# Two-token score levels, weight halves and output banks in the opening of a linear-attention and MLP kernel

## The reference

```python
f = 1.0 / (1.0 + np.exp(-f_logit))
for t in range(S):
    state = f[:, :, t, :, None] * state + np.einsum('bhd,bhe->bhde', k[:, :, t], v[:, :, t])
    y[:, :, t] = np.einsum('bhd,bhde->bhe', q[:, :, t], state)
# x = y as tokens x 384, then
xn = (x - mu) / np.sqrt(var + 1e-06) * g_ln
x = x + np.maximum(xn @ w_ch1, 0.0) @ w_ch2
# then relu(x @ w_in), a convolution over three tokens, h * sigmoid(conv), @ w_out
```

## Time and profile before

| | |
|---|---|
| median of 3 runs | 773.96 us (771.0 to 778.25) |
| the profiled execution, device time | 777.86 us |
| its span, first to last instruction | 776.1 us |
| TensorE matmul busy | 700.0 us (90%) |
| VectorE busy | 558.6 us (72%) |
| ScalarE busy | 309.0 us (40%) |
| GpSimd busy | 222.9 us (29%) |
| mean granted clock of TensorE | 0.979 |

### The profile page before, as it was taken

How to read it: one execution, slowest core, us unless ns; L and a number is a source line. 1 busy time by engine, 2 the same in 40 slices (tenths; PEclk the granted TensorE clock), 3 DMA queues, 4 the chain that set the end, 5 groups by cost and what they waited for, 6 DMA issues and landing times.

```text
span 776.1 us, 19962 instructions
## 1 busy us (share of the span) xinstructions
PE 700.0 (90%) x8672; PEld 653.0 (84%) x8672; DVE 558.6 (72%) x998; ACT 309.0 (40%) x590; POOL 222.9 (29%) x204
## 2 busy tenths in 40 slices
PE   1345689879999999999999899999989999999998
PEld 1245688779899999899899899999989999999997
DVE  6978888757776976876885886452458767767765
ACT  2353132033034134125125114212367766776764
POOL 7667632205324524434432631430000000000000
PEclk9999999789899999999999999999999999999999
DMA  8652511174134324414406220204220201201000
GB/s 249 199 164 63 113 57 49 53 154 114 52 74 150 87 55 128 129 37 140 134 3 174 59 98 32 87 17 156 89 87 1 70 20 52 71 29 42 36 36 35
DMA packets 23223, 65.82 MB, mean 85 GB/s; under 512 B 4288, under 2 KB 15296, under 8 KB 23136
## 3 DMA queue, kind: packets, MB, share of 16 engines
q1 hardware_dynamic: 23136, 64.55, 28.7%
HBM read 55.09 MB, written 9.45 MB: 83 GB/s over the span
## 4 chain that ended last, share of the span: by engine, by line
PE 59%; DVE 15%; DMA 10%; POOL 8%; issue 4%; SPq 2%; ACT 1%; DVEq 0%; POOLq 0%; ACTq 0%
DMA NEAR<-near 9%; PE bank L1145 9%; PE bank L1147 8%; PE bank L1146 8%; PE bank L952 8%; PE bank L954 7%; PE bank L953 7%; PE bank L884 6%; DVE AT L761 3%; DVE Q L738 3%; DVE TOT L732 2%; POOL NEAR L566 2%; DVE A L773 2%; POOL NEAR L581 2%; POOL NEAR L568 2%
## 5 line engine op out<-in xcount | busy, mean ns | idle before, releaser
L884 PEld LDWEIGHTS bank<-Q,K 48*64 48x64 f32 x3840 | 70.4, 151 | 52.5 <-issue 52.4
L657 ACT ACTIVATE HHI<-bank 128x384 fp32r<-128x384 f32 x96 | 47.0, 491 | 168.8 <-PE bank L954 168.6
L884 PE MATMUL bank<-Q,K 48*64 48x32 f32 x3840 | 75.3, 234 | 42.0 <-DVE Q L738 30.8
L1122 DVE SCALAR_TENSOR_TENSOR TB<-HB,CW,TB 128x440 f32<-128x440 f32 x112 | 75.8, 677 | 47.0 <-ACT TB L1085 45.0
L952 PE MATMUL bank<-HHI,W2H 128*128 128x384 f32 x288 | 105.6, 367 | 0.0
L952 PE MATMUL bank<-XH,W1H 128*128 128x384 f32 x288 | 103.3, 359 | 0.6 <-DVE XL L831 0.6
L954 PE MATMUL bank<-HHI,W2L 128*128 128x384 f32 x288 | 99.0, 344 | 0.0
L953 PE MATMUL bank<-HLO,W2H 128*128 128x384 f32 x288 | 98.7, 343 | 0.0
L953 PE MATMUL bank<-XL,W1H 128*128 128x384 f32 x288 | 97.3, 338 | 0.2 <-issue 0.2
L954 PE MATMUL bank<-XH,W1L 128*128 128x384 f32 x288 | 97.3, 338 | 0.0
L836 DVE SCALAR_TENSOR_TENSOR HLO<-bank,HHI 128x384 fp32r<-128x384 f32 x96 | 53.1, 554 | 47.1 <-ACT HHI L657 46.1
(11 more groups left out here) (116 smaller groups left out, 1443.0 us busy)
## 6 DMA issues: line engine op xcount, KB each, us to landing
NEAR<-near SPq DMA_DIRECT2D x23, 960.0 KB, 4.9
V<-v SPq DMA_DIRECT2D x8, 576.0 KB, 9.0
x2d<-X SPq DMA_DIRECT2D x8, 576.0 KB, 4.3
F<-f SPq DMA_DIRECT2D x14, 288.0 KB, 5.3
K<-k SPq DMA_DIRECT2D x14, 288.0 KB, 5.1
Q<-q SPq DMA_DIRECT2D x14, 288.0 KB, 6.6
XB<-x2d SPq DMA_DIRECT2D x6, 663.0 KB, 5.5
out<-OB SPq DMA_DIRECT2D x6, 660.0 KB, 4.4
```

Source lines behind the costliest of these rows:

```text
L657: nc.scalar.activation(HHI[:, g % RA], ub[g % 2][:, 0:T], ACT.Relu).then_inc(hh_ready, 1)
L884: ins = mm(scores[half, par, at:at + QUARTER], K[u.par][rows, c, j, half], right[:, :, 1, :], start=True, stop=True)
L1122: nc.vector.scalar_tensor_tensor(out=TB[:, g % RB], in0=HB[:, g % RB, tap:tap + TB_], scalar=CW[:, g, tap:tap + 1], in1=TB[:, g % RB], op0 ...
```

## The change

The first unit no longer uses NEAR, and the low halves of the weights no longer come from GpSimd.

- **Two-token blocks of unit 0.** `even` and `odd` are two more score levels: K with the even tokens of Q before the gates are applied, and, after K's even tokens are scaled (`baseK`), with the odd ones. `self` puts them into AT with a predicated copy. `baseK` and `baseQ` of unit 0 now wait for them. `near`, `nsum` and `neary` of unit 0 are gone, and so are three loads of 960 KB.
- **Weights.** ScalarE scales and rounds in one pass (`whi`). For the pieces 0 to 7 TensorE forms in each half of a piece (128x384) diag(g_ln) times the staged half (an fp32 product) minus the high half (an fp32r product) in one of the two banks of `up` (`wsub`), and ScalarE copies it out (`wlo`). The pieces 8 to 11 are done by VectorE in one pass (`wlv`).
- **Banks.** For unit 0 `y`, `kv` and `xnt` write the banks 0, 1 and 2, and `xadd` of unit 0 is a copy on ScalarE without an addition.
- **State.** ST has two buffers; `sscale` reads one and writes the other, and so waits for the `y` of the chunk before instead of its own.
- **Setup.** GpSimd makes one more mask (SELF) and clears AT[0] earlier and AT[1] too.
- **Order.** START and LOADS are new lists.

```diff
-        ST = attn("ST", [P, NP, 2 * D])
+        ST = [attn(f"ST{i}", [P, NP, 2 * D]) for i in range(2)]
+        NPE = 8
...
             def load_w(_, j):
                 if j >= NS:
-                    sp.wait_ge(wl_ready, j - NS + 1)
+                    if j - NS < NPE:
+                        sp.wait_ge(wp_done, 2 * (j - NS + 1))
+                    else:
+                        sp.wait_ge(wd_ready, j - NS - NPE + 1)
...
-            def weights(_, j):
-                _, hi, lo = WJ[j]
-                pool.wait_ge(wh_ready, j + 1)
-                nc.gpsimd.tensor_tensor(lo, stage(j), hi.bitcast(F32), ALU.subtract).then_inc(wl_ready, 1)
...
-                    nc.scalar.activation(stage(j), stage(j), ACT.Copy, scale=GLN[:, kt:kt + 1]).then_inc(wg_ready, 1)
-                    act.wait_ge(wg_ready, j + 1)
-                nc.scalar.copy(WJ[j][1], stage(j)).then_inc(wh_ready, 1)
+                    nc.scalar.activation(WJ[j][1], stage(j), ACT.Copy, scale=GLN[:, kt:kt + 1]).then_inc(wh_ready, 1)
+                else:
+                    nc.scalar.copy(WJ[j][1], stage(j)).then_inc(wh_ready, 1)
+
+            def wlo(_, h):
+                act.wait_ge(wp_done, h + 1)
+                nc.scalar.copy(half_of(WJ[h // 2][2], h), ub[h % 2][:, 0:DM]).then_inc(wl_ready, 1)
...
+            def wsub(_, h):
+                j = h // 2
+                if h == 0:
+                    pe.wait_ge(gd_ready, 1)
+                pe.wait_ge(wh_ready, j + 1)
+                if h > 1:
+                    pe.wait_ge(wl_ready, h - 1)
+                by = GD[:, j // (F1 // WCH)] if j < NW1 else ID[:]
+                to = ub[h % 2][:, 0:DM]
+                mm(to, by, half_of(stage(j), h), start=True, stop=False)
+                mm(to, MINUS, half_of(WJ[j][1], h), start=False, stop=True).then_inc(wp_done, 1)
...
             def baseK(p, _):
+                if u.first:
+                    dve.wait_ge(even_done[p.ahead], 1)
...
             def sscale(u, c):
-                dve.wait_ge(y_done, u.count(NC, c + 1))
-                if c or not u.first:
+                if c == (1 if u.first else 0):
+                    dve.wait_ge(prep_ready[0], u.count(PREPS, PREPS))
+                if u.index or c:
+                    dve.wait_ge(y_done, u.count(NC, c))
                     dve.wait_ge(st_ready, u.count(NC, c))
...
                     if c == 0 and u.half == 0:
-                        ins = nc.vector.memset(st, 0.0)
+                        if u.first:
+                            dve.wait_ge(const_ready, 2)
+                        ins = nc.vector.memset(to, 0.0)
...
             def up(u, g):
                 if u.first:
-                    pe.wait_ge(wl_ready, NW1)
+                    pe.wait_ge(wl_ready, 2 * NPE)
```

More of the change, by code:

```diff
@@ L309, in phase_a @@
                 "xh", "xl")
-        TREE = ("gates", "baseK", "baseQ", "pT", "pK", "pQ", "score", "mask", "copy")
+        TREE = ("gates", "even", "odd", "self", "baseK", "baseQ", "pT", "pK", "pQ", "score", "mask", "copy")
         PERIOD = steps("""
@@ L353, in phase_a @@
[L353 to L357, removed]
@@ L408, in wstage, with nears, bank_of, state @@
             return WST[j % 2][:, 0:flat].rearrange("p (a b) -> p a b", a=n)
-        def near_of(u, c):
-            return NEARS[1] if u.first and c == 1 else NEARS[0]
+        def nears(u, more):
+            return u.count(NC, more - NC)
+        def bank_of(kind, u):
+            return {"y": bank[0], "kv": bank[1], "xnt": bank[2]}[kind] if u.first else yb
+        def state(u, c):
+            return ST[(u.index * NC + c) % 2]
         def stage(j):
@@ L682, in xb @@
                     nc.scalar.copy(nxt.XBH[0][:, d], nxt.XB[0][:, d]).then_inc(nxt.xbh_ready, 1)
[L684 to L685 removed]
+            walk(act, dict(wb=wb, xb=xb, gates=gates, near=near_, copy=copy, xadd=xadd, ktok=ktok, xh=xh, hhi=hhi,
+                           xout=xout, diag=diag, whi=whi, wlo=wlo))
         def vector(dve):
@@ L849, in xb @@
                                             ALU.subtract).then_inc(nxt.xbl_ready, 1)
-            walk(dve, dict(wb=wb, xb=xb, baseK=baseK, baseQ=baseQ, pK=pK, pT=pT, pQ=pQ, mask=mask, nsum=nsum, xadd=xadd,
-                           sscale=sscale, st=st_, norm=norm, xn=xn, xl=xl, hlo=hlo))
+            walk(dve, dict(wb=wb, xb=xb, baseK=baseK, baseQ=baseQ, self=self_, wlv=wlv, pK=pK, pT=pT, pQ=pQ,
+                           mask=mask, nsum=nsum, xadd=xadd, sscale=sscale, st=st_, norm=norm, xn=xn, xl=xl, hlo=hlo))
         def tensor(pe):
@@ L862, in score @@
                 pe.wait_ge(prep_ready[p.ahead], u.count(PREPS, st + 1))
+                if st == 0 and u.first:
+                    pe.wait_ge(self_done[p.ahead], 1)
                 if st > MASKED:
@@ L888, in ktr @@
             def ktr(u, c):
-                if c:
+                if u.first and c or u.index == 1 and c == 0:
+                    pe.wait_ge(ktok_ready, u.count(NC, c))
+                elif c:
                     pe.wait_ge(st_ready if c == 1 else xl_ready, u.count(NC, 1))
@@ L901, in y @@
             def y(u, c):
-                first = c == 0 and u.half == 0
-                pe.wait_ge(ktok_ready, u.count(NC, c + 1))
+                first, to, before = c == 0 and u.half == 0, bank_of("y", u), state(u, c - 1)
+                if not u.first:
+                    pe.wait_ge(ktok_ready, u.count(NC, c + 1))
+                elif c:
+                    pe.wait_ge(x_ready, c)
                 if u.first and c == 0:
@@ L977, in down @@
                 ins.then_inc(down_done, 1)
-            walk(pe, dict(score=score, ktr=ktr, y=y, kv=kv, xnt=xnt, xacc=xacc, up=up, down=down))
+            walk(pe, dict(wsub=wsub, even=even, odd=odd, score=score, ktr=ktr, y=y, kv=kv, xnt=xnt, xacc=xacc, up=up, down=down))
         return dict(sync=sync, gpsimd=gpsimd, scalar=scalar, vector=vector, tensor=tensor), nxt
```

283 lines of the change are left out of this document (191 added, 92 removed).

## The result

| | before | after |
|---|---|---|
| median | 773.62 us (771.0 to 778.25) | 748.46 us (746.53 to 751.77) |
| span of the profiled execution | 776.1 us | 744.8 us |
| `up0.0` starts | 89.44 us | 83.75 us |
| first `xout0` (unit 0 is through) | 172.63 us | 146.33 us |

The ratio is 0.9673 [0.9613, 0.9733]. 763 was predicted with 752 as the lower end; the change brought 25 us and not 11.

The account below looks back on a forecast made before the run. VectorE, busy 73.5 of the first 90 us, was taken to hold back `up0.0`; starting it 9.0 us earlier plus 1.9 less behind gave 10.9 off 777.9, so 767.0 profiled and 763 median, range 752 to 775.

Parts of the forecast that it names:

- The collisions on VectorE: Before `up0.0`, VectorE products stretched by GpSimd's SBUF reads; four groups carry 9 us, counted as gain by unit 0's last `pQ6`.
- The list up to `up0.0`: TensorE's work from 51.6 us, half slow and half fast, ends at 80.4, above VectorE's 78.5; `up0.0` starts then.
- The reason given for the clock: Ahead of `up0.0`, full-array `wsub`, a third of TensorE's list, with hardly any idling, should raise the clock within or before it.
- Behind `up0.0` there is less to do: Behind `up0.0`, two scores of 1.60 us already done, `xacc` of at most 1.3 added: 1.9 us less.
- PERIOD and all behind it stay as they are: The order list PERIOD and everything behind it were taken as unchanged, with no gain or loss.
- (c): Rival, chance 0.07: the stretch behind `up0.0`, with 10.7 us of idle TensorE, grows by what was won; 774 us.
- (a): Rival, chance 0.22: clock rises early, between the opening's scores; `up0.0` at 73.5, gain 18, 756 us, or 752.
- 9 us before 89.4: Start of `up0.0`, the first dense product: forecast at 80.4 us, so 9 us earlier than in the kernel before.
- (b): Rival, chance 0.19: clock stays low up to `up0.0`, which starts at 90 or 94; 773 to 777 us.
- (d): Rival, chance 0.10: unhidden fp32 weight loads ahead of `wsub` add 0.6 us per half; `up0.0` at 100, 783 us.
- One sign on record for being wrong: In the opening, a `wsub` half on TensorE taking over 1.7 us was listed as showing the prediction wrong.

Follow-up runs that it names:

- e11: The kernel before, own order, with low weight halves only cleared and `near` of unit 0 left out with its sums and loads: 756.17 us, ratio 0.975.
- e9: e1 with the low weight halves cleared by GpSimd instead of subtracted, `near` of unit 0 kept: 761.03 us, ratio 0.981.
- e6: The changed kernel with the low halves of pieces 0 to 7 zeroed by GpSimd in place of `wsub` and `wlo`: 752.48 us, ratio 0.967.
- e7: e1 with low weight halves only cleared and `near` of unit 0 left out with its sums and loads: 756.18 us, ratio 0.973.
- e2: The changed kernel with the order of the kernel before from `up0.0` on: 767.80 us, ratio 0.991.
- e1: The kernel before with two state buffers and the changed kernel's order of each engine from `up0.0` on: 774.83 us, ratio 0.998.

## Why the prediction was wrong

The direction and the first cause were right; the size was less than half.

**The collisions on VectorE: right in kind, too small where they were weighed.** "The four groups alone carry ... together 9 us." They do, but they were taken for nearly the whole ("the collisions (9 and more)"). Summed over all of VectorE's rows with one instruction, each against the shortest row of its form up to 175 us, the surplus is about 20 us in the first 90 us of before and under 1 in the first 84 of after; in e11 it is 3 in the first 71. The groups by form of before have it in many small places, of which these carry another 2.4 (3 x 0.8 over the shortest, 0.47), 1.6 and 1.6 us, and a wait for `rstd` of 3.2:

```profile
L825 DVE TENSOR_SCALAR XN<-X,MV,RSTD 128x384 f32<-128x384 f32 x3 | 3.8, 1274 | 3.2 <-POOL RSTD L595 3.2
L709 DVE TENSOR_TENSOR Q<-Q,F 128x1536 f32<-128x1536 f32 x1 | 3.4, 3359 | 0.0
...
L732 DVE TENSOR_TENSOR TOT<-TOT 128x16 f32<-128x16 f32 x2 | 2.0, 978 | 0.0
```

e11 weighs GpSimd's two jobs together: 20 us of the median, with the order unchanged. That is not the collisions alone. VectorE's busy time ahead of `up0.0` falls from 73.0 to 51.2 us, some 16 of it by shorter rows and 3.5 by the sums for `near`, which are left out too; and its two waits for GpSimd, 3.2 and 1.6 us, are gone. The low halves alone (e9, with `near`, its sums and its loads in place) bring 10.4 at `up0.0`. GpSimd's clears in e11 leave the product of 128x256 at 0.424 us. The Trainium skill (SBUF — State Buffer, Who interferes with whom) says that a GpSimd instruction which only writes does not block VectorE; the trace agrees.

**The list up to `up0.0`: nearly right, by terms that cancel.** 80.4 was predicted, 83.75 came. `self` was priced 4.3 us and took 7.5 (0.75 and 1.32 us a copy, not 0.385 and 0.7): the rows of contiguous masks were carried over to copies that write every second element. A `wsub` half took 1.9 us slow and 0.89 fast, not 1.6 and 0.8. The last `pQ6` of unit 0 ended at 59.9 and not at 54, hardly before: 3.2 us of the difference are `self`, and VectorE waited 7.1 us for slow scores where 5 were allowed. From there it needed 23.4 us to the last `xl` (to 83.4), where 22 and 2.5 for collisions were allowed. TensorE was back at the full rate at 60 us, where the prediction had it only half way through its list, at 71; that made up for the dearer halves, and both engines were ready together. So the near hit at `up0.0` is luck. The reason given for the clock does not hold: it was to rise by the `wsub` in the list, and in e6 it rises at the same point without any.

**The step that failed: "Behind `up0.0` there is less to do ... so 1.9 less", "PERIOD and all behind it stay as they are".** The moved work was credited with TensorE's time for it, two scores at 1.60 less `xacc`. But the stretch behind `up0.0` in before was not all TensorE's own work. It had 10.7 us of idle TensorE, and the clock at 0.90 was worth another 8.3, an estimate (a tenth of 83.2). Both go with the first levels of unit 1's tree between the dense products: e11, which has them there, is idle 8.9 us at 0.92, and e7, which has them ahead and the new order behind, 0.8 us at 1.00. Their place alone is not enough: e2 has the scores 1 and 2 ahead and the old order behind, and is idle 14.2 us at 0.88. TensorE's waits of before, 90 to 173 us, and of after, 84 to 147:

```profile
PE bank L884 <- issue: 4.9, 2, 3.8
PE bank L877 <- DVE Q L738: 1.6, 1, 1.6
PE bank L915 <- ACT KTOK L645: 1.4, 2, 0.7
```

```profile
PE bank L1004 <- issue: 0.8, 1, 0.8
PE bank L1092 <- ACT W2L L708: 0.7, 1, 0.7
PE bank L997 <- DVE Q L797: 0.5, 2, 0.3
```

With the tree three levels further on at `up0.0` and the new order behind it, the idle time falls from 10.7 to 1.2 us (9.5) and the low clock goes (8.3); less work is the rest, 2.8. That is the 20.6. The prediction saw both items and set them aside: rival (c) named the 10.7 us only as something that might grow, and (a) gave half of the clock's 8 us to a case of its own.

Yet e7 and e11 show that a stretch shorter by as much need not be a gain. With the same work left out of both, the order that takes 17.7 us off the stretch is worth nothing at `xout0`: it only puts the opening's gain behind `up0.0` (e7) and not ahead of it (e11). e2 shows the other side: once the opening has done unit 1's first levels, the old order behind it gives 22.8 us away at `xout0`, against after. The price of the new opening with unit 1's steps ahead is e1 against after: 106.3 to 83.75, 22.5 us, where the prediction had "9 us before 89.4". Of these 22.5, GpSimd's two jobs carry 17.1 (e1 to e7); the place of the two scores is in the rest. So the error is one error: an opening that was relieved of some 20 us by GpSimd's jobs and then given some 10 us of unit 1's work on VectorE was credited only with what was left at `up0.0`.

**The 5 us of after over e11.** After does all the work that e11 leaves out, with TensorE's and ScalarE's help, and is still 4.9 us ahead at `xout0`. The own banks and `xadd` on ScalarE, which the prediction priced at nothing, may carry it, or the clock from 60 us on, or the place of the scores 1 and 2: in e7 TensorE waits 12.7 us for them, in after not. None of the three was undone by itself, so this stays open.

**The rivals.** (b) and (d) did not come: the clock rose at 60 us. The 0.6 us more for a half in (d) came from no row; a slow half took 1.9 us in all, 0.3 over its price. (a), 756, was nearest, though its condition was not met (26 to 60 us stayed slow). (c) was the opposite of what happened. One sign on record for being wrong did come, a half at over 1.7 us, but it was not what the time turned on.

## What to carry to other kernels

When a change moves work past the mark by which you measure, compare at a mark behind both, or price the kernel before with the moved work added; the mark's own shift says nothing. Sum a contention over all of an engine's rows and not over the groups that stand out: here the top four held 9 of some 20 us. When a copy or a product is priced from another row, take one with the same access pattern; its elements alone missed by a factor of 1.8.

## What the runs showed of the hardware

**Short runs in a target.** A predicated copy whose target and mask lie at every second element took 1.316 us for 64x512 and 0.748 for 64x256; with neighbours in turn for both 0.728 and 0.439, although the bank was then read with a stride of 32 elements. These runs do not part the target from the mask; the copies of `mask`, whose mask is read without gaps at each level, speak for the target: at the first level, whose target runs are two elements long, two copies of 64x256 took 1.29 us, at a later level 0.77. VectorE's timeline of after, three copies of `self` and two masks of the first level:

```profile
22.46 3.80 DVE L767 COPY_PREDICATED AT<-KTOK,bank 64x512 f32<-64x512 int32 x3
...
29.07 1.29 DVE L820 COPY_PREDICATED AT<-MASK,bank 64x256 f32<-64x256 int32 x2
```

The Trainium skill (SBUF — State Buffer, Door 1: The DMA port swizzle) says that fp32 may be strided by up to 4 elements for free; these rows speak against it for VectorE's predicated copy, in the target as far as `mask` tells.

**The row of the granted clock** can read 1.00 at the start whatever the rate, as if it had no entry yet: e11 has 1.00 in every stretch up to 64 us, and yet its whole-unit score at 55.7 us takes 2.79 us. Only durations tell the rate there.

**A short burst lifted the clock, a long busy stretch did not.** In after three `wsub` halves in a row take 1.65, 1.48 and 0.81 us for the fp32 product, at 19.6, 21.3 and 22.8 us: the rate doubles within them. TensorE then stands still for 2.5 us; from 26 us it is at 1.2 GHz again and stays there to 60, although TensorE is busy 12.0 of the last 12 us of that:

```profile
19.57 1.65 PE L949 MATMUL bank<-X,XN 128*128 128x384 f32 x2
...
21.33 1.48 PE L949 MATMUL bank<-X,XN 128*128 128x384 f32 x2
...
22.84 0.81 PE L949 MATMUL bank<-X,XN 128*128 128x384 f32 x2
```

```profile
48.00:60.00 12.00, 12.00 (x217) 8.93 (x213) 8.69 (x20) 8.42 (x21) 0.00 (x0) 0.50 0.12 36
```
